# Moving attention and router steps to other sites in a hand-written software pipeline

## The reference, cut to what matters

```python
# 1: attention in chunks of 32 queries, each against 8 memory keys and a window of 56
a = softmax(scale * q_c @ k_full.T);  x = a @ v_full          # -> x [3072, 512]
# 2: a dense layer
h = x @ w_in;  g = h * cos(h);  x = g @ w_out                 # 512 -> 2048 -> 512
# 3: a router and one of eight experts for each row with x @ w_skip > 0
e = argmax(x @ w_gate);  gate = max(softmax(x @ w_gate))
out = x + gate * (relu(x @ w1[e]) @ w2[e])                    # other rows: out = x
```

## Time and profile before

| what | value |
|---|---|
| time, median of 3 | 877.95 us (877.71 to 879.40) |
| the profiled execution: time, span | 877.95 us, 876.3 us |
| PE busy in the span | 819.5 us (94%), mean granted clock 0.973 |
| DVE busy | 520.9 us (59%) |
| ACT busy | 469.0 us (54%) |
| chain that ended last | PE 87%, DVE 5%, ACT 2%, DMA 2%, issue 2% |

### The profile page before, as it was taken

The page is one execution under the profiler, slowest core; times in us unless marked ns, Lnnn a source line. Parts: engine busy times, 40 slices in busy tenths (PEclk is TensorE's granted clock), DMA queues, the critical chain, the costliest instruction groups (busy, mean ns, idle before and its releaser), DMA issues.

```text
span 876.3 us, 20405 instructions
## 1 busy us (share of the span) xinstructions
PE 819.5 (94%) x8018; PEld 725.3 (83%) x8019; DVE 520.9 (59%) x1030; ACT 469.0 (54%) x809; POOL 50.2 (6%) x57
## 2 busy tenths in 40 slices
PE   5799999999999999999999999999982989999995
PEld 3688888898888888888888888898961878999994
DVE  3677655655565655556555655654458577666664
ACT  3577665565566555555655565563461555444442
POOL 0000000000000000000000000000014022111110
PEclk9799999999999999999999999999995899999998
DMA  9822031104213210422132031020053375655653
GB/s 337 298 82 68 25 109 62 61 25 134 65 58 106 65 61 27 119 76 61 60 111 61 26 108 62 25 73 1 1 195 89 128 279 193 215 201 224 231 205 118
DMA packets 40690, 97.42 MB, mean 111 GB/s; under 512 B 5852, under 2 KB 5852, under 8 KB 40608
## 3 DMA queue, kind: packets, MB, share of 16 engines
q1 hardware_dynamic: 37632, 90.21, 30.3%
q0 software_dynamic: 2976, 6.05, 1.9%
HBM read 82.34 MB, written 16.79 MB: 113 GB/s over the span
## 4 chain that ended last, share of the span: by engine, by line
PE 87%; DVE 5%; ACT 2%; DMA 2%; issue 2%; POOL 0%; SPq 0%; POOLq 0%; DVEq 0%; ACTq 0%
PE h_ps L721 30%; PE y_ps L735 29%; PE h_ps L822 9%; PE y_ps L837 7%; PE s_ps L625 2%; PE s_ps L662 2%; PE turn L686 1%; PE turn L676 1%; DMA xg<-x_mid,idx_from 1%; PE turn L640 1%; DMA k_pre<-qk 1%; PE turn L696 1%; DVE w_lo L1262 1%; PE turn L807 1%; PE s_ps L807 0%
## 5 line engine op out<-in xcount | busy, mean ns | idle before, releaser
L721 PE MATMUL h_ps<-xT_hi,in_hi 128*128 128x384 f32 x512 | 181.5, 354 | 1.7 <-DVE xT_lo L1067 1.4
L721 PE MATMUL h_ps<-xT_hi,in_lo 128*128 128x384 f32 x512 | 173.5, 339 | 0.0
L721 PE MATMUL h_ps<-xT_lo,in_hi 128*128 128x384 f32 x512 | 173.0, 338 | 0.0
L735 PE MATMUL y_ps<-out_hi,g_hi 128*128 128x512 f32 x384 | 150.0, 391 | 5.0 <-DVE g_lo L1144 5.0
L735 PE MATMUL y_ps<-out_hi,g_lo 128*128 128x512 f32 x384 | 152.1, 396 | 0.0
L735 PE MATMUL y_ps<-out_lo,g_hi 128*128 128x512 f32 x384 | 151.6, 395 | 0.0
L901 ACT ACTIVATE hs<-h_ps 128x384 f32<-128x384 f32 x128 | 62.5, 488 | 156.1 <-PE h_ps L721 155.9
L1138 DVE TENSOR_SCALAR whole<-us 128x384 f32<-128x384 f32 x128 | 45.3, 354 | 131.8 <-ACT us L902 131.8
L925 ACT ACTIVATE us<-us 128x384 f32<-128x384 f32 x128 | 67.2, 525 | 73.2 <-DVE us L1140 72.9
L721 PEld LDWEIGHTS h_ps<-xT_hi,in_hi 128*128 128x128 f32 x512 | 97.2, 190 | 5.3 <-DVE xT_lo L1067 1.8
L721 PEld LDWEIGHTS h_ps<-xT_lo,in_hi 128*128 128x128 f32 x512 | 97.4, 190 | 1.6
(11 more groups left out here) (156 smaller groups left out, 1209.3 us busy)
## 6 DMA issues: line engine op xcount, KB each, us to landing
raw<-w SPq DMA_DIRECT2D x72, 512.0 KB, 5.6
k_sb<-qk SPq DMA_DIRECT2D x22, 512.0 KB, 4.5
v_sb<-v SPq DMA_DIRECT2D x22, 512.0 KB, 3.5
x_mid<-x SPq DMA_DIRECT2D x24, 256.0 KB, 5.2
out<-x SPq DMA_DIRECT2D x24, 256.0 KB, 5.6
q_sb<-qk SPq DMA_DIRECT2D x22, 256.0 KB, 3.1
in_raw<-w_in SPq DMA_DIRECT2D x4, 1024.0 KB, 14.0
out_raw<-w_out SPq DMA_DIRECT2D x4, 1024.0 KB, 15.0
```

What stands on the lines that cost most here:

```text
L721: last = pe.matmul(h_ps[:, f % 2, 0:BN], w[:, dc, f * P:(f + 1) * P], x[:, half, dc, :], start=(n == 0), stop=(n == 3 * DC - 1))
L735: last = pe.matmul(y_ps[:, j, :], g[:, f % RING, j * P:(j + 1) * P], w[:, f, :], start=(f == 0 and n == 0), stop=(f == FT - 1 and n == 2))
```

## The change

It changes two lists of site numbers. For each attention tile, scores, exp and sum move one site earlier (scores from 5, 13, 21 to 4, 12, 20; exp from 6, 14, 22 to 5, 13, 21; sum from 8, 16, 24 to 7, 15, 23). The probs, values and x steps keep their sites (9, 11, 13 for the first tile). In the router the last logits step moves from site 27 to 23, route from 28 to 24, rexp from 29 to 25 and gate from 30 to 26. No instruction is added or removed by the source, and all buffers and waits stay.

```diff
 ATTENTION = []
-for _j, _b in enumerate((5, 13, 21)):
-    ATTENTION += [(_b, "scores", _j), (_b + 1, "exp", _j), (_b + 3, "sum", _j), (_b + 4, "probs", _j),
-                  (_b + 6, "values", _j), (_b + 8, "x", _j)]
+for _j, _b in enumerate((4, 12, 20)):
+    ATTENTION += [(_b, "scores", _j), (_b + 1, "exp", _j), (_b + 3, "sum", _j), (_b + 5, "probs", _j),
+                  (_b + 7, "values", _j), (_b + 9, "x", _j)]
 ROUTER = [(5, "x1", 0), (7, "logits", 0), (11, "x1", 1), (15, "logits", 1), (19, "x1", 2),
-          (27, "logits", 2), (28, "route", 0), (29, "rexp", 0), (30, "gate", 0)]
+          (23, "logits", 2), (24, "route", 0), (25, "rexp", 0), (26, "gate", 0)]
```

## The result

The changed kernel takes 883.43 us (881.10 to 884.52, 8 runs) against 878.57 us before, measured together: a ratio of 1.0059 with a 95% interval of 1.0045 to 1.0074. That is 4.9 us slower; 882.6 had been forecast. The profiled execution took 885.1 us with a span of 883.4 us, so it lies above all eight of these, and its 7.1 us over the span of before must not be read as the cost of the change.

A forecast was written before the change was run, and what follows sets the result against it. PE was taken to bound the full blocks, ACT and DVE to set the pace in block 0. Terms +3.1 + 0 + 1.3 + 0.6 - 0.3 = +4.7 on 877.95 gave 882.6 us, with 879.0 to 886.0 expected 8 times in 10.

The forecast's parts named there:

- Term 1: Block 0: the Exp and its table load land ahead of take_h, making g_lo and later downs late; +3.1 us.
- Term 2: Full blocks 1 to 6: no new PE wait, with about 0.7 us left on the tightest bank; 0 us.
- Term 3: PE's borders: last logits standing alone in blocks 1 to 6, +1.3 us; scores parted from x at 20 places, +0.6.
- Term 4: End of block 7: earlier rexp takes the Sin load off the last cosine's path; -0.3 us.
- (a): Rival: taking the Exp off block 0's g chain wins, both 1.4 us holes go, 875.9 us; chance 0.07.
- (b): Rival, no change: block 0 loses only the first tile's 0.9 us, PE's borders cost nothing, 878.5 us; chance 0.10.
- (c): Rival: full blocks break, logits 1 and 2 wait 0.5 us for the bank in six blocks, 888.6 us; chance 0.05.
- (d): Rival: block 0's holes bring the clock to 1.2 GHz for some 10 us, 887.6 us; chance 0.04.

The follow-up runs named there:

- attention part alone: Kernel before with only the attention list moved (scores, exp, sum one site earlier), router at its old sites: 881.41 us, ratio 1.0026.
- exp back: Changed kernel with exp returned to sites 6, 14, 22 in block 0 only, scores and sums staying early: 880.65 us, ratio 1.0011.
- router part alone: Kernel before with only the router's last logits, route, rexp and gate moved, attention at its old sites: 888.14 us, ratio 1.0092.
- memset later: Changed kernel with GpSimd's iotas and memsets after the blocks waiting for the last fraction of block 7: 883.12 us, ratio 1.0035.
- changed again: The changed kernel itself, timed again on one chip with the kernel carrying both repairs: 884.48 us, ratio 1.0055.
- router with the sum: Kernel before with the router's steps moved and the third tile's sum moved to site 23: 882.21 us, ratio 1.0024.
- block 0 on old sites: Changed kernel with block 0 walking the old attention sites, all other blocks the new ones: 881.94 us, ratio 1.0032.
- the two with early sums: Kernel before with block 0's sums one site earlier: 876.10 us, ratio 0.9959; and the same with w_in's split pieces also moved: 875.43 us, 0.9949.
- spread split: Kernel before with block 0's sums one site earlier and w_in's split pieces 3 to 7 at f = 1, 5, 7, 9, 11: 875.43 us, ratio 0.9949.

## Why the prediction was right, and where it was not

**Term 1, the Exp ahead of take_h (+3.1 forecast, +3.44 measured; attention part alone +3.40).** The steps came as walked, with 0.15 us to be added to the times after for the earlier start: take_h(3) 46.98 forecast, 46.84 measured; g_lo(2) 49.57 and 49.45; cosine(3) 50.65 and 50.54; down(3) 55.25 and 55.13; down(6) 71.8 and 71.66; down(7) 76.85 and 76.73; down(10) 93.55 and 93.61. Holes of 7.6 us were forecast and 6.8 are shown. The rest of the loss is in PE's busy time, which grew from 74.68 to 75.81 us. That is the four more holes again: the up ahead of a hole counts 2.27 us instead of 2.11 (46.18 to 48.45, where the hole before down(2) begins; 46.08 to 48.19 before), and the down behind it 2.18 instead of 2.05 (50.05 to 52.23; 48.19 to 50.24), which for four holes makes about 1.2. The walk had counted the holes alone. With the exp back alone the loss goes.

**Term 2, no new wait in full blocks: right, and its margins too.** The longest waits there are unchanged at 0.2 us. In block 2 the room between g_lo(2), g_lo(6) or g_lo(10) and its down grew by 1.49, 0.75 and 1.12 us (0.8 to 1.4 forecast). On the bank, the transposes of x at 222.55 us were followed by ACT's copy at 225.26, by DVE's subtraction until 226.57 and by the logits at 227.27, so the forecast 0.7 us were left. That this held because the sum moves along with route I had not seen; the router part alone opened six holes of 0.40 to 0.57 us. I had weighed route at its new site with the sum already at its own, and never asked what the one would do without the other.

**Term 3, PE's borders.** The logits were right: 1.3 forecast, 1.24 measured. The parted scores were forecast at 0.6 for 20 places and measured at 0.34 for the 18 in blocks 1 to 6; the value taken from the matmuls of values was the right end of the range. The second is hardly more than what blocks 1 to 6 vary by between executions, some 0.3 us.

**Term 4, the end of block 7 (-0.3 forecast, +0.96 measured): the step that failed.** "What is next is the down itself" looked at ACT and PE alone. Moving gate also took away POOL's last DMA, which had held the memset back, and the memset then held back DVE's fraction for 1.45 us. The saving itself was real: 0.5 us with the memset out of the way. The Trainium skill has a rule for this in "SBUF — State Buffer", section "Who interferes with whom": GpSimd and a VectorE `tensor_scalar` in a two-port mode take a shared pair of ports in turn, whoever starts first, while a `tensor_tensor` meets only GpSimd's reads. No row says in which mode this TENSOR_SCALAR ran, but the traces agree with the rule: it ended 0.36 us after the memset's end (649.58 + 1.82 against 649.24 + 1.80), and the TENSOR_TENSORs beside the memset, in the kernel with the memset later, kept 0.56 us.

**The sum** was 4.7 forecast; the profile shows 5.8 up to the experts (term 1 0.3 too small, term 4 off by 1.3, term 3 0.5 too large), and the medians moved by 4.9. What lies between 5.8 and 4.9 was not settled: single executions of one kernel differ by more. The mechanism of block 0, the largest part, was foreseen, but that 882.6 came within 0.8 us of 883.43 is in part luck: a missed loss of 1.3 us was offset by 0.5 too much in term 3 and by what the medians moved less than the stages.

**The rivals.** (a) would have decided at a take_h(3) before 45.0, and it started at 46.84. (b) fell with the second and third tile's holes. (c), a wait on the bank in full blocks, did not come. (d), a fall of the clock in block 0, did not come in the changed kernel's profile, whose scores fill the first hole in part, but it did in three others.

## What to carry to other kernels

In a software pipeline with several in-order engines a step costs what stands behind it on its engine, so the same move can be free where the engine idles and dear where it sets the pace: walk the one stage that has holes and price the saturated ones by the spacing of the busy engine's own instructions. Test the parts of a rearrangement one at a time, but expect them not to add up, for one may carry the cover of the other. When a step that feeds a queue moves earlier, ask what on that queue was being held back by it, GpSimd's idle-looking memsets included.

## What the runs showed of the hardware that was not expected

- A TENSOR_SCALAR of 128x384 elements took 1.82 us instead of 0.36 when it began inside a GpSimd memset of 1.80 us, in all six profiles with the early gate and no delay of the memset (changed, changed again, router alone, router with the sum, block 0 on old sites, exp back). It did not in the two with the memset delayed, nor in the four with the old router sites (before, attention alone, and the two with early sums).
- PE's granted clock fell from 2.4 to 1.2 GHz in block 0 of three profiles, around the first wait for g_lo: for 6.8 us with a wait of 2.65 us (old block 0), and for 3.4 us after waits of 2.16 (router with the sum) and 1.96 us (spread split). In the nine others that wait was 0.97 to 1.87 us and the clock stayed up. At the end of block 7, after the wait of 1.80 us, it fell for 3.4 us in three kernels (router alone, exp back, old block 0) and stayed up in the three others with the same wait, so the length of a wait alone does not decide it. The row is of the router part alone, its last downs:

```profile
655.00:658.00 3.00, 3.00 (x9) 2.32 (x8) 0.36 (x1) 0.00 (x0) 0.00 (x0) 0.50 1.01 399
```

  There the last two downs took 5.96 us, against 4.39 in the changed kernel's profile (652.52 to 656.91). Which executions it strikes is open, as there is one profile of each.
